# Attention with hashed buckets: the column sums of v taken on DVE before the ones products

## The reference

```
mask = q_bucket[:, :, :, None] == k_bucket[:, :, None, :]
scores = scale * np.matmul(q, k.transpose(0, 1, 3, 2))
scores = np.where(mask, scores, -1000000000.0)
scores = scores - np.max(scores, axis=-1, keepdims=True)
attn = np.exp(scores)
attn = attn / (np.sum(attn, axis=-1, keepdims=True) + 1e-09)
return np.matmul(attn, v).astype(np.float32)
```

## Time and profile before

| | |
|---|---|
| median of 3 runs | 740.07 us (739.12 to 744.24) |
| the profiled execution: its own time, its span | 739.32 us, 737.5 us |
| PE busy over the span | 90%, 6360 products |
| DVE, ACT, POOL busy | 48%, 40%, 55% |
| share of the chain that ended last | PE 81%, DVE 7%, POOL 4% |
| products L604 and L605 | 96 and 96, from 29.6 us to 204.9 us |
| attention stage | from the start to about 216 us |

### The profile page before, as it was taken

The page is one execution under the profiler, slowest core; times in us unless marked ns, Lnnn a source line. Parts: engine busy times, 40 slices in busy tenths (PEclk is TensorE's granted clock), DMA queues, the critical chain, the costliest instruction groups (busy, mean ns, idle before and its releaser), DMA issues.

```text
span 737.5 us, 14841 instructions
## 1 busy us (share of the span) xinstructions
PE 664.9 (90%) x6360; PEld 435.3 (59%) x6370; DVE 354.7 (48%) x621; ACT 298.6 (40%) x487; POOL 402.4 (55%) x231
## 2 busy tenths in 40 slices
PE   3899999999989129999999787999999999999995
PEld 0366666666679139999998673444444444444442
DVE  5888888888541726544556642422322223223221
ACT  1555565556644006676667824322121111221112
POOL 4576787768759581788989982623122111131112
PEclk8899999999985559999999779999999999999998
DMA  6886676757624164676878990000001000010001
GB/s 183 185 188 165 126 171 149 173 105 151 234 65 165 62 240 156 230 255 246 299 234 287 347 335 1 0 1 1 0 1 58 0 1 1 0 58 1 0 1 57
DMA packets 47073, 90.96 MB, mean 123 GB/s; under 512 B 16448, under 2 KB 20672, under 8 KB 47008
## 3 DMA queue, kind: packets, MB, share of 16 engines
q1 hardware_dynamic: 45088, 83.71, 38.9%
q0 software_dynamic: 1920, 6.31, 2.2%
HBM read 76.72 MB, written 6.30 MB: 113 GB/s over the span
## 4 chain that ended last, share of the span: by engine, by line
PE 81%; DVE 7%; POOL 4%; DMA 3%; ACT 2%; issue 1%; SPq 1%; DVEq 0%; ACTq 0%; POOLq 0%
PE psum L780 9%; PE psum L782 9%; PE psum L781 8%; PE psum L797 4%; PE psum L796 4%; PE psum L798 4%; PE psum L556 4%; PE psum L570 4%; PE psum L571 3%; PE psum L712 3%; PE psum L714 3%; PE psum L713 3%; PE psum L731 3%; PE psum L733 3%; PE psum L732 3%; PE psum L590 2%
## 5 line engine op out<-in xcount | busy, mean ns | idle before, releaser
L1255 POOL TENSOR_TENSOR low<-ring 128x4096 bf16<-128x4096 f32 x20 | 140.1, 7014 | 38.4 <-DMA ring<-in_moe_w 32.0
L1300 POOL TENSOR_TENSOR s_lo<-sv,s_hi 128x512 bf16<-128x512 f32 x36 | 42.0, 1166 | 213.6 <-ACT s_hi L818 213.6
L1235 POOL TENSOR_TENSOR probs_lo<-probs 128x768 bf16<-128x768 f32 x80 | 117.9, 1488 | 57.5 <-ACT probs L843 57.0
L843 ACT ACTIVATE probs<-psum 128x384 f32<-128x384 f32 x192 | 91.6, 491 | 65.5 <-PE psum L571 63.7
L780 PE MATMUL psum<-y,ring 128*128 128x512 bf16 x288 | 109.8, 381 | 4.1 <-DVE sv L1201 4.1
L782 PE MATMUL psum<-y,low 128*128 128x512 bf16 x288 | 109.9, 382 | 0.0
L781 PE MATMUL psum<-y,ring 128*128 128x512 bf16 x288 | 109.7, 381 | 0.0
L1193 DVE TENSOR_TENSOR gp<-psum,inv_at 128x512 f32<-128x512 f32 x36 | 24.9, 691 | 146.6 <-PE psum L782 145.6
L981 DVE TENSOR_REDUCE psum<-psum 128x1 f32<-128x768 f32 x96 | 87.8, 960 | 14.3 <-PE psum L556 14.0
L926 ACT ACTIVATE sig<-gp 128x512 f32<-128x512 f32 x36 | 22.7, 630 | 136.4 <-DVE gp L1193 136.4
L731 PE MATMUL psum<-hT,ring 128*128 128x0 bf16 x320 | 68.1, 233 | 4.0 <-POOL low L1255 4.0
(11 more groups left out here) (189 smaller groups left out, 1482.9 us busy)
## 6 DMA issues: line engine op xcount, KB each, us to landing
ring<-in_moe_w SPq DMA_DIRECT2D x20, 2048.0 KB, 8.9
pair_in<-in_qk SPq DMA_DIRECT2D x8, 768.0 KB, 4.8
head<-in_qk SPq DMA_DIRECT2D x16, 384.0 KB
head<-in_qk SPq DMA_DIRECT2D x32, 192.0 KB, 5.0
head<-pair_in SPq DMA_DIRECT2D x32, 192.0 KB, 4.0
rows_in<-sorted_x SPq DMA_DIRECT2D x12, 257.0 KB, 4.5
value<-in_v SPq DMA_DIRECT2D x16, 192.0 KB, 5.6
ring<-in_moe_w_gate SPq DMA_DIRECT2D x4, 768.0 KB, 12.1
```

The source lines that it names most:

```text
L843: nc.scalar.activation(probs[h % 2][:, t, half * HALF:(half + 1) * HALF], bank(ST_BANK + n % 2)[:, 0:HALF], ACT.Exp, scale=SCALE).then_inc ...
L1235: G.tensor_tensor(probs_lo[par][:, t, :], probs[par][:, t, :], probs_up[par][:, t, :], ALU.subtract)\
L1255: G.tensor_tensor(low[k % RING][:, :], ring[k % RING][:, :], upper[k % RING][:, :, 1], ALU.subtract)\
```

## The change

For each head DVE adds the six key tiles of v into one row of 65 numbers per partition, in fp32 (`sum_keys`: one reduction of 6x65 numbers that it reads with a step of 65 words, then one subtraction of 65 numbers that makes the low part). `value_sum` on PE then takes two products instead of twelve. `sum_keys(0)` stands ahead of the loop, behind `query_low(1)`; `sum_keys(h+1)` stands last in head h. PE's wait for `value_lo_ready` moves from `value_sum` to `weigh_values`.

```diff
+        key_sum = [sb(f"key_sum{i}", [P, UW], F32, at) for i in range(2)]
+        key_sum_lo = [sb(f"key_sum_lo{i}", [P, UW], BF16, at) for i in range(2)]
...
                     pe.wait_ge(plo_dve_ready, h + 1)
+                    pe.wait_ge(value_lo_ready, h + 1)
                     pe.wait_ge(vsum_ready, h + 1)
...
             def value_sum(h):
 
-                b = h % BUFS
-                pe.wait_ge(value_lo_ready, h + 1)
+                pe.wait_ge(keys_summed, h + 1)
                 o = bank(T_BANK)[:, HALF:HALF + UW]
-                for kt in range(T):
-                    mm(o, ones[:, :], value_up[b][:, kt, :], start=(kt == 0), stop=False)
-                    last = mm(o[:, 0:D], ones[:, :], value_lo[b][:, kt, :], start=False, stop=(kt == T - 1))
-                last.then_inc(sum_ready, 1)
+                mm(o, ones[:, :], key_sum_up[h % 2], start=True, stop=False)
+                mm(o, ones[:, :], key_sum_lo[h % 2][:, :], start=False, stop=True).then_inc(sum_ready, 1)
...
+            def sum_keys(h):
+
+                b = h % BUFS
+                dve.wait_ge(value_in[b], 16 * (h // BUFS + 1))
+                if h >= 2:
+                    dve.wait_ge(sum_ready, h - 1)
+                own.link(V.reduce_sum(key_sum[h % 2][:, :], value[b][:, :, :].rearrange("p t c -> p c t"), AX.X))
+                V.tensor_tensor(key_sum_lo[h % 2][:, :], key_sum[h % 2][:, :], key_sum_up[h % 2], ALU.subtract)\
+                    .then_inc(keys_summed, 1)
...
             query_low(1)
+            dve.wait_ge(heads_zeroed, 2)
+            sum_keys(0)
...
                 if h == hash_slot(p) and p < PAIRS:
                     signs(p)
                     query_low(p)
+                if h + 1 < NH:
+                    sum_keys(h + 1)
```

More of the change, by code:

```diff
@@ L262, in build @@
         value_up = [x[:, :, :].bitcast(BF16).rearrange("p t (n two) -> p t n two", two=2)[:, :, :, 1] for x in value]
+        key_sum_up = [x[:, :].bitcast(BF16).rearrange("p (n two) -> p n two", two=2)[:, :, 1] for x in key_sum]
         wo_up = wo[:, :, :].bitcast(BF16).rearrange("p j (n two) -> p j n two", two=2)
@@ L315, in build @@
         sum_ready = sem("sum_ready")
+        keys_summed = sem("keys_summed")
         vsum_ready = sem("vsum_ready")
```

## The result

The changed kernel took 753.09 us (median of 4 runs, 749.79 to 758.59) against 740.48 for the kernel before: a ratio of 1.017, 95% interval 1.0099 to 1.024. The profiled execution took 753.07 us, its span 751.3.

A forecast was written before the change was run, and what follows sets the result against it. PE bounds the attention stage, but behind hash heads DVE sets the end. Terms -4.65 + 9.7 + 1.05 + 0.5 = +6.6 us, plus 4.8 for the clock, on 739.3 give 750.7, by the median some 751; range 740.5 to 756.

The forecast's parts named there:

- The stall behind hash heads: PE's wait for DVE behind six hash heads grows from 0.76 to 2.38 us, the subtraction waiting for POOL: +9.7 us.
- two witnesses: L974 and L1030, DVE subtractions of two SBUF tiles, taking 2.30 for 1.04 and 1.53 for 0.96 us beside POOL.
- no wait for POOL: Rival: the small subtraction slips in beside POOL, normalisation 0.97 us late behind hash heads only; 740.8 us; chance 0.23 (740 to 744).
- The clock: Drops, 3.41 us stretches of PE at 1.2 GHz, follow three of the six long stalls, 1.6 us each: +4.8 us.
- one row: The profile's single PE pause of such length, 2.13 us idle from 207.65, followed by 3.41 us at half clock.
- The reduction: DVE's stepped reduction of 390 numbers takes 0.82 us, or 0.56 if the step costs nothing.
- the row of 96 stepped numbers: L1097, a reduction of 96 numbers read with a step, 316 ns; gives 1.7 ns a number.
- The other heads: Behind seven heads without hash products, 1.14 us of cover is used up with 0.15 left over each: +1.05 us.
- The start: sum_keys(0) and sum_keys(1) at the start cost between 0 and 1.8 us; 0.5 taken.
- the cover that I had named: At the start, POOL's queue covers sum_keys(0), so 0.5 us is taken from the range 0 to 1.8.
- PE: Ten products fewer save 0.31 us a head, lost in head 0, kept in fifteen heads: -4.65 us.

The follow-up runs named there:

- one SBUF input: Changed kernel with the subtraction exchanged for a maximum over one element each, reading one SBUF tile instead of two: 741.19 us, ratio 1.0011.
- the kernel with the reduction early: Changed kernel with the reduction behind DVE's fourth row-maximum reduction and the subtraction on POOL: 734.58 us, ratio 0.9936; once more 736.14 us, ratio 0.9934.

## Why the prediction was right

*The stall behind hash heads.* Forecast 2.38, from POOL's end plus 0.1; measured 2.36, ending 0.08 to 0.09 after POOL. The step rested on two witnesses with 768 numbers, and the question was whether 65 would wait alike. They do, in fifteen heads of sixteen, and "one SBUF input" with L1022 shows it is the inputs. The rival "no wait for POOL" gave 740.8; the kernel in which there was no wait measured 741.19, so the price of that rival was about right and its condition was not met. The page "SBUF — State Buffer", section "Who interferes with whom", of the Trainium skill says that a reduction never contends with GpSimd on trn2; the trace agrees, with 0.834 to 0.868 us for the sixteen reductions, of which nine began while POOL ran.

*The clock.* Forecast three drops, measured four, at 1.55 us each for the 1.6 taken. With one row to go by, that drops would come was a judgement; the pause put into the kernel before showed that the stall alone brings them. Their number was no forecast at all but the middle between none and six, and that it fell so near is luck. Without its four drops the changed kernel would stand near 747, so they are half of the loss of 12.6 us between the medians; set against the drop that the kernel before had at the end of the stage, the clock's part of the 13.76 us is 4.7, a third. The four executions of the changed kernel spread from 749.79 to 758.59 us, and the fastest has the highest mean clock, 0.945 against 0.929 to 0.931 in the others; only the first has a trace in which drops can be counted.

*The reduction.* Forecast 0.82 from the row of 96 stepped numbers, measured 0.85, and 0.55 in order, forecast 0.56.

*The other heads.* Forecast 0.15 of stall each, measured 0.30, 1.0 us in sum. The mis-sized term is the 0.12 by which the normalisation was to overlap the subtraction: there it starts 0.03 after the subtraction's end (114.28 to 114.31), and only behind hash heads 0.08 before it. Why it overlaps in the one place and not in the other, no run shows.

*The start.* Forecast 0.5 in a range of 0 to 1.8, measured 1.3. Nothing covered `sum_keys(0)`, which took 0.85 and 0.23 us with no wait for POOL: the six row maxima behind it came 1.0 us later, and PE stood in head 0 where it had not before.

```profile
27.60 0.51 PE L560 MATMUL psum<-head 96*128 96x384 bf16 x2 [0.80 <-DVE psum L983]
```

That is 1.0 of the 1.3. `sum_keys(1)` met POOL's queue, its subtraction took 1.41 us, and PE's wait for DVE at 37.88 (1.12 us idle) took the place of the 0.84 us that PE had waited anyway; this is the other 0.3. So the cover that I had named, POOL's queue, hid most of `sum_keys(1)` and nothing of `sum_keys(0)`.

*PE.* -4.65 forecast and borne out: 0.06 in place of 0.37 us a head.

In sum, the profiled executions differ by 13.75 us for a forecast of 6.6 + 4.8 = 11.4. The other heads' 1.05, the start's 0.8, the drops' 1.4 and 0.7 us of a later first hash product, which has nothing to do with the change, come to 3.95 too much; the drop at the stage's end that didn't come takes 1.5 back, and the stalls 0.1. The median came out at 753.1 for 751. The mechanism was right term by term; that the total came so near owes something to errors that cancelled.

## What to carry to other kernels

An instruction has the price of its place in an engine's queue. The same reduction of 0.83 to 0.85 us cost PE nothing between two row-maximum reductions, and 0.75 us a time ahead of the one for which PE waits; the small subtraction behind it, held by POOL, brought that to 1.60 and let the clock fall. Before DVE gets a small subtraction of two SBUF tiles, look at what POOL runs at that moment; its remaining time is the price, not the 0.2 us of the subtraction. And PE pauses of 1.9 to 2.4 us often cost more than their length here (23 drops behind 36 of them), while twelve pauses of 1.5 and 1.77 cost that alone.

## What the runs showed of the hardware

Behind stalls of 1.5 and 1.77 us PE's clock held twelve times of twelve; behind 1.9 us it fell four times of six; behind 2.36 fourteen times of eighteen, each time for 3.4 us, at some 1.5 us apiece by the account above. These are profiled executions, one for each kernel. The counts are small, so how sharp the step between 1.77 and 1.9 is stays open. The wait of 2.29 us at the end of the stage, the same in all kernels, had a drop behind it in five of twelve profiled executions (that of before among them, that of the changed kernel not), so the same pause goes both ways, and less often down than the shorter 1.9 us within the heads. Length alone doesn't decide it; what else does, these runs don't show.

Where DVE's two-input subtraction waited for POOL, it ended 0.084 to 0.088 us after POOL's instruction, in 37 cases of three kernels (fifteen, fifteen and seven), whatever its own start was.

POOL is held by DVE too. Its low part took 1.66 us beside DVE's subtraction of 768 numbers in the changed kernel, and 1.47 by itself. The subtraction of 65 numbers took 0.30 us on POOL against 0.23 on DVE, and 1.01 in head 0 of the kernel with the reduction early, beside DVE's L1047.
